# Attention, a dense FFN and a routed FFN on one core: a scatter moved behind the next gather, one loop over tile pairs, and a later place for the output rows

## What is computed

```python
# 1. attention: B, H, S, D = 4, 8, 576, 64; heads 0-3 see the last 32 positions,
#    heads 4-7 the earlier positions of the same class modulo 32
attn = softmax(where(mask, q @ k.T / sqrt(D), -1e9)) @ v
x = attn.transpose(0, 2, 1, 3).reshape(2304, 512)
# 2. dense FFN, d_ff = 2048
h = x @ w_in
x = (h * sigmoid(1.702 * h)) @ w_out
# 3. routed FFN: 8 experts, 512 -> 1024 -> 512, one expert a token, some tokens skip it
out = x.copy()
do_compute = x @ w_skip > 0
e_idx, gate_w = argmax and its softmax weight of x @ w_gate
for e in range(8):
    mask = do_compute & (e_idx == e)
    out[mask] = x[mask] + gate_w[mask] * (relu(x[mask] @ w1[e]) @ w2[e])
```

## Time and profile before

| | |
|---|---|
| three runs | 718.73, 722.6, 723.05 us; median 722.6 |
| the profiled execution | 723.05 us, span of its trace 721.4 us |
| granted TensorE clock over the span | 0.986 of full speed |
| stage 3 on PE, tile by tile (start of its first up projection) | 519.2, 555.0, 577.4, 602.2, 626.8, 651.5, 666.9, 691.8; end 707.4 us |

### The profile page before, as it was taken

One profiled execution on the slowest core, in us unless ns is written; L12 is line 12 of the kernel. 1 busy time (PEld: TensorE's weight loads), 2 busy tenths in 40 slices (PEclk: granted clock), 3 DMA queues, 4 the chain that ended last, 5 costly groups with the idle time before them and its releaser, 6 DMA issues.

```text
span 721.4 us, 14266 instructions
## 1 busy us (share of the span) xinstructions
PE 675.0 (94%) x4569; PEld 586.9 (81%) x4570; DVE 393.2 (55%) x1363; ACT 368.8 (51%) x1034; POOL 158.7 (22%) x206
## 2 busy tenths in 40 slices
PE   3889999999999999999999999999978699999992
PEld 3568888888888899998999999989866588887871
DVE  4867765555565343343442533446566676657765
ACT  4887766556565433333233333344426575566663
POOL 5344322222231010010010100101122433213431
PEclk9999999999999999999999999999999899999997
DMA  7547534223321422002011020022217775567743
GB/s 264 183 142 257 193 111 159 72 73 130 102 78 50 149 72 84 6 1 88 1 31 58 0 87 0 0 76 83 73 36 263 253 240 173 162 221 242 263 167 105
DMA packets 48219, 85.65 MB, mean 119 GB/s; under 512 B 7618, under 2 KB 11714, under 8 KB 48160
## 3 DMA queue, kind: packets, MB, share of 16 engines
q1 hardware_dynamic: 43664, 79.20, 33.4%
q0 software_dynamic: 3952, 4.65, 2.1%
q10 hardware_dynamic: 544, 1.05, 0.4%
HBM read 70.84 MB, written 18.52 MB: 124 GB/s over the span
## 4 chain that ended last, share of the span: by engine, by line
PE 85%; DVE 4%; DMA 3%; issue 2%; ACT 2%; POOL 2%; SPq 0%; POOLq 0%; ACTq 0%; DVEq 0%
PE px L1337 28%; PE ph L1324 27%; PE pe_h L1420 8%; PE py L1446 8%; PE pscore L1274 3%; PE pctx L1296 3%; PE ptrans L1283 3%; PE ph L1354 2%; DMA xg<-x_dram,gather_slots 2%; DVE w_lo L932 1%; PE phT L1432 1%; PE pxT L1400 1%; PE ph L1348 1%; DMA w_raw<-wf 1%; POOL probs L646 1%
## 5 line engine op out<-in xcount | busy, mean ns | idle before, releaser
L1324 PE MATMUL ph<-x_hi,w_hi 128*128 128x256 f32 x576 | 165.1, 287 | 1.3 <-DVE x_lo L993 1.3
L1088 DVE SCALAR_TENSOR_TENSOR gated<-gated,ph 128x256 f32<-128x256 f32 x144 | 60.5, 420 | 189.7 <-ACT gated L830 189.6
L1324 PE MATMUL ph<-x_lo,w_hi 128*128 128x256 f32 x576 | 160.5, 279 | 0.0
L1324 PE MATMUL ph<-x_hi,w_lo 128*128 128x256 f32 x576 | 160.3, 278 | 0.0
L830 ACT ACTIVATE gated<-ph 128x256 f32<-128x256 f32 x144 | 55.0, 382 | 123.3 <-PE ph L1324 123.3
L1337 PE MATMUL px<-w_hi,g_hi 128*128 128x512 f32 x288 | 117.7, 409 | 0.0
L1337 PE MATMUL px<-w_hi,g_lo 128*128 128x512 f32 x288 | 113.6, 394 | 0.0
L1337 PE MATMUL px<-w_lo,g_hi 128*128 128x512 f32 x288 | 113.0, 392 | 0.0
L1324 PEld LDWEIGHTS ph<-x_hi,w_hi 128*128 128x128 f32 x576 | 108.2, 188 | 5.4 <-DVE x_lo L993 1.5
L1324 PEld LDWEIGHTS ph<-x_lo,w_hi 128*128 128x128 f32 x576 | 108.7, 189 | 4.0
L1324 PEld LDWEIGHTS ph<-x_hi,w_lo 128*128 128x128 f32 x576 | 108.7, 189 | 0.0
(11 more groups left out here) (193 smaller groups left out, 1114.0 us busy)
## 6 DMA issues: line engine op xcount, KB each, us to landing
w_raw<-we SPq DMA_DIRECT2D x72, 256.0 KB, 3.5
more_raw<-we SPq DMA_DIRECT2D x72, 256.0 KB, 4.4
w_raw<-wf SPq DMA_DIRECT2D x32, 256.0 KB, 3.9
vs<-vw SPq DMA_DIRECT2D x16, 384.0 KB, 3.3
qs<-qT SPq DMA_DIRECT2D x16, 288.0 KB, 3.6
ks<-kT SPq DMA_DIRECT2D x16, 288.0 KB, 4.1
xT_dram<-x_stage SPq DMA_DIRECT2D x16, 288.0 KB, 2.8
x_lo<-xT_dram SPq DMA_DIRECT2D x8, 512.0 KB, 4.1
```

The lines of the kernel that those rows point to most:

```text
L1088: nc.vector.scalar_tensor_tensor(gated[s % 2][:, :], gated[s % 2][:, :], 1.0, ph[s % 2][:, 0:TT], ALU.add, ALU.mult).then_inc(gated_done, 1)
L1324: last = nc.tensor.matmul(ph[f % 2][:, 0:TT], up_w(w, k, f), x[p][:, k, :], start=(at == 0 and n == 0), stop=(at == KD - 1 and n == 2))
```

## The change

1. `MAXT` becomes (2304 + 7*255) // 256 + 1 = 16, and `T1` 18.
2. `pairs_of_tiles` writes one loop over pairs 1 to 7 in place of the two. A round whose pair does not exist is run through with its body skipped. For POOL (`after=1`) the test is one tile wider, and one conditional scatter stands behind the loop.
3. On POOL, `scatter(t - 1, 1)` moves from the end of tile t-1 behind `gather(t + 1)` of tile t. The last one is run by the round of the pair after the last tile.
4. On DVE, for all tiles but tile 0, `both_rows` moves from before chunk 9 to behind chunk 13 of the next tile's weights.

```diff
--- before.py
+++ after.py
@@ -57,8 +57,7 @@
 FPO = CH // P
 EUPCH = KD * EF // CH
 ECH = 2 * EUPCH
-MAXT = (N + P + (E - 1) * (ET - 1)) // ET + 1
-MAXT += MAXT % 2
+MAXT = (N + (E - 1) * (ET - 1)) // ET + 1
 T1 = MAXT + 2
 ROWS = E * N
 NOROW = 1 << 20
@@ -156,21 +155,14 @@
     return nullcontext() if isinstance(t, int) and t == 0 else eng.If(total > t)
 
 
-def pairs_of_tiles(eng, total, body):
+def pairs_of_tiles(eng, total, body, after=0):
 
     for p in range(2):
         body(0, p, p)
-
-    def some(pairs):
-        with eng.Fori(*pairs) as s:
-            with eng.If(total > s * 2):
-                for p in range(2):
-                    body(s, p, s * 2 + p)
-
-
-    some((1, E // 2))
-    with eng.If(total > E):
-        some((E // 2, MAXT // 2))
+    with eng.Fori(1, MAXT // 2) as s:
+        with eng.If(total > s * 2 - after):
+            for p in range(2):
+                body(s, p, s * 2 + p)
 
 
 def wait(eng, sem, value):
@@ -729,16 +721,23 @@
             load_slots(scatter_slots_of[0], 0, scatter_slots_in[0])
 
             def routed_tile(s, p, t):
+                first = isinstance(t, int) and t == 0
                 with if_exists(pool, total, t):
                     gather(t + 1, 1 - p, s + p)
+                if not first:
+                    with if_exists(pool, total, t - 1):
+                        scatter(t - 1, 1, 1 - p, s + p - 1)
+                with if_exists(pool, total, t):
                     pool.wait_ge(gathered[p], (s + 1) * 16 * EH)
                     load_slots(gather_slots[p], row_of(t + 2), gather_slots_in[p])
-                    wait(pool, rows_stored[1 - p], (s + p) * 16 * EH)
+                    if not first:
+                        pool.wait_ge(rows_stored[1 - p], (s + p) * 16 * EH)
                     load_slots(scatter_slots_of[1 - p], row_of(t + 1), scatter_slots_in[1 - p])
                     scatter(t, 0, p, s)
-                    scatter(t, 1, p, s)
-
-            pairs_of_tiles(pool, total, routed_tile)
+
+            pairs_of_tiles(pool, total, routed_tile, after=1)
+            with pool.If(total > MAXT - 1):
+                scatter(MAXT - 1, 1, (MAXT - 1) % 2, (MAXT - 1) // 2)
 
             with pool.If(total > 1):
                 pool.wait_ge(rows_stored[1], (total >> 1) * (16 * EH))
@@ -1253,8 +1252,9 @@
                     next_lo(6, 7, 8)
                     xe_split_lo(t + 1, 1 - p)
                     split_h_lo(t, 1, 1)
+                    next_lo(9, 10, 11, 12, 13)
                     both_rows()
-                    next_lo(9, 10, 11, 12, 13, 14, 15)
+                    next_lo(14, 15)
 
             pairs_of_tiles(dve, total, routed_tile)
```

## The result

The changed kernel takes 728.1 us (median of six runs, 726.68 to 730.04); beside it the kernel before took 721.97 us (718.37 to 723.3). The ratio is 1.0105, with a 95% interval of 1.0076 to 1.0135. I had forecast 720.8 us. So the change costs 6 us by the medians and 7.6 by the ratio, where I saw a gain of 2.

A forecast was written before the change was run, and what follows sets the result against it. PE, with 85% of the chain, was taken as the bound, only its stage 3 gaps and the end movable. Gains of 5.6 us against costs of 3.8 gave -1.8 us, 720.8 us; range for 8 in 10: 716.5 to 724.6.

The forecast's parts named there:

- the costing of edit 1: DVE's tables shrink from 160 to 144 elements, shortening its instructions in the chain to `meta`; 0.1 us saved.
- Tile 2's gather: Stage 3, tile 2: second gather issued 2.80 us earlier, PE's gap falls from 5.5 to about 2.65 us; 2.8 us saved.
- The clock: Stage 3, tile 2: with the shorter gap PE's clock no longer falls behind it; all 1.6 us come back.
- Tile 6: Stage 3: the gather starts 0.6 us earlier, which takes away PE's 0.5 us wait; 0.5 us saved.
- Tile 7's `relu`: Stage 3's last tile: weight chunks load earlier, so ACT's `relu` no longer waits behind a late one; 0.6 us saved.
- The rows behind five subtractions: Tile 7, DVE: five `w_lo` now stand before the output rows, delaying everything after them; +3.0 us.
- POOL's tail: End of POOL: branches between the last two scatters cost 0.3 us, empty rounds before its final waits 0.5; +0.8 us.
- Rival (e): PE's jumps over the loop body in empty rounds take 5.11 us each; about 741 us; chance 0.03.
- (a): Tile 2's gather lands no earlier because the DMA engines' backlog sets the landing; 725.2 us; chance 0.11.
- Rival (b): PE's clock falls in tile 2's shorter gap as well, 1.6 us less gained; 722.4 us; chance 0.12.
- Rival (c): POOL's 5.96 us drain swallows some of the 3.8 us added at the end; down to 717.0 us; chance 0.12.
- (d): Empty rounds at the end cost POOL more than SP's price, +2 us; 722.8 us; chance 0.08.

The follow-up runs named there:

- after_moved320: The changed kernel, short tables kept, with 320 unused bytes in front of `fill_rows` so stage 2 and 3 buffers have their old addresses; ratio to the kernel before 0.9984.
- after_tables20: The changed kernel with T1 back at 20, so the tables have their old length and later buffers their old addresses; 721.29 us, ratio to the kernel before 1.0001.
- before_rows_late: The kernel before with only `both_rows` moved behind chunk 13; 723.88 us, ratio to the kernel before 1.0031.
- before_again: The kernel before, unchanged, run for a second profile; 718.6 us.
- after_tables20_rows_early: The changed kernel with T1 back at 20 and `both_rows` back in front of chunk 9; 718.9 us, ratio to the kernel before 0.9966.

## Why the prediction was wrong

The step that failed is the sentence that the change "touches only stage 3, so nearly all of the time is out of its reach", and with it the costing of edit 1 by DVE's instructions alone (-0.1 us). Shorter tables move all buffers behind them, and the matmuls of both FFN stages depend on where their operands lie against each other. Price: 728.1 - 720.5 = 7.6 us by the medians against the same kernel with its buffers put back (`after_moved320`), 8.7 by the two ratios (1.0105 and 0.9984). By the rows, from the first matmul of the gate's logits in stage 2 to the start of stage 3 it took 396.0 us (126.9 to 522.9) and 390.0 with the buffers put back (128.5 to 518.5), and the long tiles of stage 3 took up to 0.4 us more each. No row of the trace of before could have given this price; the rival should have been there all the same, since the diff changes the size of a buffer.

What is left of the forecast is -1.8 us. `after_moved320` lies at 0.9984 (-2.9 to +0.5 us by its interval), which allows it, and `after_tables20` at 1.0001 (-1.0 to +1.2), which doesn't. So the rest was right in kind and too hopeful in size. Its parts, one by one:

- Tile 2's gather, -2.8 us by the issue. Right in kind (the second gather went out 3.4 us before PE was ready for it, 568.71 against 572.1, where it had been 0.9), too large in size. From the tick behind `scatter(0, 0)` to the second gather it was 5.32 us before (560.08 to 565.40) and is 3.10 now (565.61 to 568.71): 2.2 and not 2.8, because the long tick (1.57 and 1.56 us) is now the gather's own. The wait fell by 1.6 by the middle values. I had read the slowest of the profiles as the rule.
- The clock, -1.6 us. The eight transposes of tile 2's input take 1.09 us at the full clock. With the moved scatter they took that in three of five profiles, 1.46 in one and 1.90 in one; without it in three of eleven. So the loss became rarer and did not go, and the term is some part of 1.6 us. My argument from the 2.66 us before 539.20 was wrong, as `before_rows_late` shows.
- Tile 6, -0.5: the wait is gone, but not for my reason. From the transposes of the tile before to the second gather it was 11.39 us before (645.24 to 656.63) and is 11.18 now (646.50 to 657.68), 0.2 sooner and not 0.6; and with edit 4 alone, where nothing on POOL was moved, the wait was gone as well, by a faster landing. The number came out by luck.
- Tile 7's `relu`, -0.6: from the end of PE's up projection to DVE's first `h_lo` it took 1.81 us in the profile before (697.47 to 699.28) and 1.16 after (698.55 to 699.71). But in `before_again` it took 1.15 (693.71 to 694.86), and about that in every other profile with early rows. The loss stood in my one profile alone, and there was nothing to win.
- The rows behind five subtractions, +3.0: measured 3.04 in this profile. In the four profiles with five subtractions before the last rows the time from the first `h_lo` to the rows was 12.1 to 12.9 us, in the eleven others that keep all the last tile's work 9.1 to 9.6. By the medians of `after_tables20` and `after_tables20_rows_early` late rows cost 2.4.
- POOL's tail, +0.8: with early rows 0. With late rows the last scatter's DMA starts 3.9 us after the rows begin (711.86 to 715.74) in place of 3.4, since the first one's took 1.88 us and not 1.29; the landing, 2.16 in place of 2.43, gave 0.3 of that back. `before_rows_late`, with the old loop, has the same 1.89 us, so this comes with the late rows and not with the branches. I should have let POOL's work cover its sequencer.

With these sizes (-1.6, none to all of -1.6, -0.5, 0, +3.0, +0.2) the sum lies between +1.1 and -0.5 us, where the two kernels lay at 0 and -1.2.

Rival (e), far branches: the loop's branches on PE took at most 0.22 us each, whether back (L162) or over a skipped body (L163), and the one of 5.11 us has no counterpart. By the Trainium skill ("Runtime: NRT & Kernel Launch", instruction fetch mechanics) a taken branch forces a fetch only when its target lies outside the window held; in these rounds no branch took long enough to be one. How large that window is, no run here shows.

Of the rivals (a) gave the number nearest to the result (725.2), for a reason that the profile refutes: the gather did land earlier against PE's work. Rival (b), a fall of the clock in the shorter gap, came true in two of the five profiles with the moved scatter. Rival (c) did not: the drain was as long as before. Nor did (d).

## What to carry to other kernels

A change of a small buffer's size is a change of every address behind it; before the time of an edit is read, look whether stages that it does not touch kept their pace, and if not, put the addresses back with padding and measure again. A gain read from one profiled wait on a DMA needs a second profile: the same wait here ran from 2.3 to 5.5 us, and the late weight chunk of tile 7 held up the end in one profile only. Work for a step that does not exist (the weights of a tile past the last) is free only as long as nothing on the last path stands behind it.

## What the runs showed of the hardware

With unchanged instructions, full clock and no idle time, stage 2's up-projection matmuls of 128x256 fp32r, whose weights and input lie 192 bytes apart modulo 256, followed each other every 116 ns (1.397 us for 12), and at distances of 0 or 128 every 120 ns (1.442 to 1.445). That is 3.4% on such matmuls and 1% on the kernel, and at these distances each tile of stage 2 took the same time to 0.04 us. The Trainium skill says of TensorE's path to SBUF that it never waits on anyone ("SBUF — State Buffer", SBUF: two separate sides). That is said of contention between engines, and no run here contradicts it there; but how fast PE's own matmuls followed each other depended here on the addresses of their operands. What in the chip makes it so, no run shows. A POOL drain of 5.95 us stood at the end of all sixteen profiles, whatever came before it.
